# Turning moved ahead of the value products on TensorE, the whole copy ahead of the exponential on ScalarE

## What is computed

```python
scores = scale * np.matmul(q, k.transpose(0, 1, 3, 2))
thresh = np.max(scores, axis=-1, keepdims=True) - tau
scores = np.where(scores >= thresh, scores, -1000000000.0)
attn = np.exp(scores - np.max(scores, axis=-1, keepdims=True))
attn = attn / (np.sum(attn, axis=-1, keepdims=True) + 1e-09)
x = np.matmul(attn, v)             # then, heads side by side:
x = (h * np.tanh(softplus(h))) @ w_out    # h = x @ w_in
x = (h * clip(h + 3, 0, 6) / 6) @ w_out2  # h = x @ w_in2
```

## Time and profile before

| | |
|---|---|
| median of 3 runs | 1116.96 us (1115.6 to 1117.17) |
| the profiled execution, its own time | 1116.74 us |
| its span in the trace | 1115.0 us |
| attention stage | the first 310 us or so |
| PE busy | 1098.8 us, 99% of the span |
| VectorE busy | 423.6 us, 38% |
| ACT busy | 489.9 us, 44% |
| POOL busy | 263.5 us, 24% |

### The profile page before, as it was taken

The page is one execution under the profiler, slowest core; times in us unless marked ns, Lnnn a source line. Parts: engine busy times, 40 slices in busy tenths (PEclk is TensorE's granted clock), DMA queues, the critical chain, the costliest instruction groups (busy, mean ns, idle before and its releaser), DMA issues.

```text
span 1115.0 us, 15233 instructions
## 1 busy us (share of the span) xinstructions
PE 1098.8 (99%) x6064; PEld 880.3 (79%) x6064; DVE 423.6 (38%) x903; ACT 489.9 (44%) x882; POOL 263.5 (24%) x179
## 2 busy tenths in 40 slices
PE   6999999999999999999999999999999999999998
PEld 5767676767668888889988888888888888888897
DVE  6878887878831211112121112123223223222222
ACT  5778787877743332223232234442233233232232
POOL 6686558556621300000000015430000000000000
PEclk9999999999999999999999999999999999999999
DMA  7432223223022000000000022300010010010010
GB/s 221 132 108 65 77 74 97 65 66 96 11 76 76 1 1 1 1 1 1 1 1 1 19 75 96 96 18 1 1 38 1 1 38 0 1 39 1 1 39 20
DMA packets 42488, 46.09 MB, mean 41 GB/s; under 512 B 3504, under 2 KB 30128, under 8 KB 42416
## 3 DMA queue, kind: packets, MB, share of 16 engines
q1 hardware_dynamic: 42416, 45.10, 13.6%
HBM read 40.37 MB, written 4.72 MB: 40 GB/s over the span
## 4 chain that ended last, share of the span: by engine, by line
PE 97%; DVE 1%; ACT 1%; issue 1%; DMA 0%; SPq 0%; DVEq 0%
PE banks L489 35%; PE banks L462 12%; PE banks L464 12%; PE banks L463 12%; PE banks L409 8%; PE banks L356 7%; PE banks L368 5%; PE banks L364 3%; PE banks L389 2%; DVE probs L709 0%; DVE neg_max L725 0%; ACT exps L572 0%; DMA q_raw<-qT 0%; ACT probsT L537 0%; DVE totals L741 0%
## 5 line engine op out<-in xcount | busy, mean ns | idle before, releaser
L770 DVE SCALAR_TENSOR_TENSOR g_low<-gate,g_high 128x512 fp32r<-128x512 f32 (+1 forms) x160 | 102.7, 642 | 473.2 <-ACT g_high L645 473.2
L462 PE MATMUL banks<-x_low,w_in_high 128*128 128x512 f32 (+1 forms) x640 | 235.9, 369 | 0.0
L463 PE MATMUL banks<-x_high,w_in_low 128*128 128x512 f32 (+1 forms) x640 | 235.5, 368 | 0.0
L464 PE MATMUL banks<-x_high,w_in_high 128*128 128x512 f32 (+1 forms) x640 | 235.5, 368 | 0.0
L645 ACT ACTIVATE g_high<-gate 128x512 fp32r<-128x512 f32 (+1 forms) x160 | 94.3, 589 | 309.6 <-PE banks L489 309.1
L462 PEld LDWEIGHTS banks<-x_low,w_in_high 128*128 128x128 f32 x640 | 120.6, 188 | 21.2 <-issue 0.6
L463 PEld LDWEIGHTS banks<-x_high,w_in_low 128*128 128x128 f32 x640 | 120.6, 188 | 20.5
L464 PEld LDWEIGHTS banks<-x_high,w_in_high 128*128 128x128 f32 x640 | 120.7, 189 | 20.0
L725 DVE TENSOR_REDUCE neg_max<-banks 128x1 f32<-128x576 f32 x144 | 108.7, 755 | 50.3 <-PE banks L356 50.1
L489 PE MATMUL banks<-g_low,w_out_high 128*128 128x512 f32 (+1 forms) x320 | 118.0, 369 | 0.8 <-issue 0.8
L489 PE MATMUL banks<-g_high,w_out_low 128*128 128x512 f32 (+1 forms) x320 | 117.8, 368 | 0.0
(11 more groups left out here) (59 smaller groups left out, 1430.1 us busy)
## 6 DMA issues: line engine op xcount, KB each, us to landing
q_raw<-qT SPq DMA_DIRECT2D x64, 144.0 KB, 2.8
k_raw<-kT SPq DMA_DIRECT2D x64, 144.0 KB, 2.8
w_in_raw<-w_in SPq DMA_DIRECT2D x16, 512.0 KB, 4.3
w_out_raw<-w_out SPq DMA_DIRECT2D x16, 512.0 KB, 4.7
out<-x SPq DMA_DIRECT2D x18, 256.0 KB, 2.9
values<-v SPq DMA_DIRECT2D x16, 256.0 KB, 3.1
values<-v SPq DMA_DIRECT2D x16, 32.0 KB, 2.8
tau_in<-tau SPq DMA_DIRECT2D x1, 0.5 KB, 2.8
```

Of the source, the lines that this page charges most:

```text
L462: nc.tensor.matmul(bank, w_in_high[:, t, cols], low, start=(t == 0), stop=False)
L463: nc.tensor.matmul(bank, w_in_low[:, t, cols], high, start=False, stop=False)
L464: mm = nc.tensor.matmul(bank, w_in_high[:, t, cols], high, start=False, stop=(t == KT - 1))
L770: nc.vector.scalar_tensor_tensor(out=g_low[:, f % 2, 0:width], in0=gate[:, f % 2, 0:width], scalar=1 / 6 if layer_of(c) else 1.0, in1=f32( ...
```

## The change

In PE's `attention_step` the call of `turn` moves from the end to a place ahead of `spread_sums` and `mix`, right behind `score_tile`. In ACT's `attention_step` `keep_main` moves from behind the exponential to a place ahead of it, right behind `keep_tail`. The waits inside the functions stay as they are. VectorE's, POOL's and SP's programs are the same.

```diff
@@ PE attention_step @@
                 pair, b = it * PAIRS_IT + p - 1, (p + 1) % 2
+                if (not first or s >= 2) and (ahead or s < 2):
+                    turn(t - 2, (s - 2) % TILES_IT)
                 if not first or p == 1:
                     if i in (2, 3):
                         spread_sums(pair, b, i - 2)
...
                 if not first and i in (0, 1):
                     mix(it, pair - 1, 1 - b, 1, part1[i])
-                if (not first or s >= 2) and (ahead or s < 2):
-                    turn(t - 2, (s - 2) % TILES_IT)
@@ ACT attention_step @@
                 if (not first or s >= 2) and (ahead or s < 2):
                     keep_tail(t - 2, (s - 2) % TILES_IT, it * PAIRS_IT + (s - 2) // PAIR_TILES)
+                if (not first or s >= 2) and (ahead or s < 2):
+                    keep_main(t - 2, (s - 2) % TILES_IT)
                 if ahead:
                     act.wait_ge(max_ready, t + 1)
...
-                if (not first or s >= 2) and (ahead or s < 2):
-                    keep_main(t - 2, (s - 2) % TILES_IT)
```

## The result

The changed kernel takes 1163.14 us (four runs, 1162.98 to 1163.21) against 1116.98 us (1115.6 to 1117.17): 1.0416 times, with a 95% interval of 1.0398 to 1.0434. That is 46.2 us slower. The forecast was 1147 us, so its sign and place were right and its size was two thirds of what came (30.2 of 46.2 us).

The account below looks back on a forecast made before the run. PE, busy nearly throughout, was taken to bound the kernel, so its stalls in attention add one for one: 9.5 + 9.7 + 11.0 = 30.2 us on 1116.74 gives 1147 us, range 1132 to 1167 (own range 1138 to 1160).

Parts of the forecast that it names:

- (a): Steps 6 to 7: turning waits for weigh, queued behind scale_mixed on VectorE; 0.63 us in 15 pairs, 9.5 us.
- (b): Steps 1 to 2: turning waits for weigh behind the 320-column scale_mixed; 0.69 us in 14 pairs, 9.7 us.
- (c): Steps 2 to 4: scores wait for keep_tail behind the spread copy, main transposes for keep_main; 0.73 us, 15 pairs, 11.0 us.
- switches: Gaps between kinds of PE matmul around product blocks: value 0, bounds -0.09 to +0.13 us a step (-12 to +18 us).
- rival 1: Both ends of each product block: early weight loads save 0.22 us a step; 1117 or 1106 us; chance 0.06.
- (d): The other steps: weigh lets PE go at 1.65 us, PE returns at 1.90; no stall, cover 0.25 us.
- (e): The first pair and the end of attention: 0 us for the two together, from -2 to +1 us.
- Rival 2: Attention steps: ACT is not late, so only (a) and (b) appear; 1136 us; chance 0.15.
- Rival 3: Turning into product has the whole 0.22 us as gap, or (d)'s cover breaks by 0.3 us; 1165 us; chance 0.13.
- Rivals 1 and 4: The fourth: waits on scale_mixed shorter than read, ACT's hidden, front gap of product blocks saved; 1124 us; chance 0.06.

Follow-up runs that it names:

- The copy late: The changed kernel with the copy of the spread factors moved behind keep_tail and keep_main in ACT's queue: 1145.23 us, ratio 1.0255 to the kernel before.
- scale_mixed late: The changed kernel with scale_mixed moved behind weigh and the threshold in VectorE's queue: 1145.1 us, ratio 1.0255 to the kernel before.
- with the addition left out on both sides: Addition of 1e-9 to the row sums (L741) left out of the changed kernel, 1162.13 us, and of scale_mixed late, 1139.86 us.
- the run with both moves and no addition: The changed kernel with scale_mixed behind weigh, the spread copy behind keep_main, and the addition of 1e-9 (L741) left out: 1121.87 us, ratio 1.0054.
- ACT's half alone: The kernel before with only keep_main moved ahead of the exponential on ACT, PE as before: 1116.7 us, ratio 1.0002.
- scale_mixed late without the addition: The changed kernel with scale_mixed behind weigh and the addition of 1e-9 to the row sums (L741) left out: 1139.86 us, ratio 1.0212.

## Why the prediction was right in kind and short in size

Per pair the forecast was 30.2 / 15 = 2.0 us, the period shows 3.10 us. By the forecast's own steps, read from start to start, for the pair from 202.94 to 225.11 us of the changed kernel:

| step of the forecast | forecast, us a pair | measured |
|---|---|---|
| (a) turning waits in step 7 | 0.63 | 0.70 |
| (b) turning waits in step 2 | 0.69 | 0.75 |
| (c) scores wait for keep_tail, step 3 | 0.47 | 0.46 |
| (c) the same, step 4 | 0.25 | 0.25 |
| (c) main transposes wait for keep_main | 0.08 | 0.14 |
| (c) wait that was there before | -0.07 | -0.07 |
| restarts after the five waits | 0 | 0.41 |
| switches, nine steps | 0 | 0.46 |
| sum | 2.05 | 3.10 |

**The waits.** (a) and (b) were right in their releases: 1.39 us after the products' end was forecast and measured, and for (a) 1.33 and 1.33. What was off is the other side of the subtraction, the time at which PE comes back. I put 0.70 us for the scores, which is their length up to a product. Ahead of a turning they take 0.64, so PE came sooner and waited more. The 0.06 us that the switch saves in front went straight into the stall. (c) was right to 0.01 in both halves of the scores' wait. Its third part is 0.14 us where 0.08 was put: bank 6 was given as free at 1.41 us, though 0.79 + 0.57 is 1.36 and the text names nothing for the other 0.05; it was let go at 1.45 (207.57 to 209.02). The experiments bear the table out once restarts are added to the bare waits. The copy late should give 0.85 + 0.27 = 1.12 us a pair, 16.8 us in 15, and with the 0.16 us of every second pair some 18; 17.9 came. scale_mixed late should give 1.45 + 0.14 = 1.59 us a pair, some 23 us; with the addition left out on both sides 22.3 came (1162.13, then 1139.86), with it 18.

**Restarts,** a term that was missing. After a wait for keep_tail the next score matmul follows 0.24 us later and not 0.13 (208.40 to 208.64): 0.11 twice. A turning that waited takes 0.70 us up to the next block and not 0.63 (206.29 to 206.99): 0.07 twice, and 0.05 after the main transposes' wait. A wait on PE costs its length and then the start of a new group. The kernel before showed it for scores: behind the ones at 21.28 the next started at 21.52, 0.24 later, and I took only the release from that row. The turning at 25.30 can't show it, since its main transposes waited too.

**The switches** were the term with bounds of -0.09 and +0.13 us a step and 0 as its value. The turning costs 0.11 more ahead of a product, where 0.09 was put. The scores cost 0.06 less, where 0.09 was counted: the gap behind them shrinks from 0.22 to 0.14, but the first one takes 0.24 to the next behind a product where it was 0.22. Together 0.05 a step by the rows, 5.6 us by the run with both moves and no addition. The sign that I had named for a mis-sized switch, a distance from the turning to the product far from 0.45 us, did not say from which transpose: it is 0.63 from the first and 0.52 from the second. Why the boundary costs what it does stays open. The weight row ahead of the products shows 0.17 us idle for issue after a turning too (214.47), so rival 1, in which loads are drawn ahead there, did not come. By the rule of the Trainium skill (TensorE: Matmul & The Clock Gate, Part 2) such loads are drawn ahead when the row groups don't conflict or when they go to the background buffer; by that rule, the trace doesn't agree at this switch, unless neither condition holds there, which no run here shows.

**The cover of (d)** held for weigh, thin as it was: in the changed kernel steps 8, 0 and 1 are 0.05 or 0.06 us longer each and no more, and so is step 5 in every second pair. In the others it is 0.21 us longer, by keep_main and not by weigh. It is the cover of weigh that the collision with POOL breaks when scale_mixed stands late. (e) was about right: the spreading of the first pair starts 0.55 us later (28.45, then 29.00), within the bounds given; the other half of it, the end, was not read apart.

**The rivals.** Rival 2, ACT not late, fell with the waits for L553 and the 18 us that the later copy gives back. Rival 3 came near by its time (1165 us) but for another reason: not one dear switch but small terms in all nine steps, restarts among them. Rivals 1 and 4 did not come. That 1163 us lie inside the range of 1132 to 1167 is in part luck: they lie above the forecast's own 1138 to 1160, and the range reaches higher only for rival 3, whose mechanism was not the one.

None of the versions of this order that were run beats the kernel before. With the waits taken out of it 5.6 us are left for the switches.

## What to carry to other kernels

When a block on a full engine is moved, reckon each consumer from a common point: when is its data released, what stands ahead of it in its queue, and when does the full engine come back for the result. The danger is a small instruction that waits for the moved block (scale_mixed, the spread copy) with something urgent queued behind it; moving that one behind the urgent work gave back 38 of 46 us here. Give each wait on PE its restart as well, and take the length of a block up to the block that will really follow it.

## What the runs showed of the hardware

A nine-column SBUF-to-SBUF addition on VectorE (L741) takes 0.16 or 0.17 us alone. Where it comes while a POOL operation on SBUF has some time to run it lasts until 0.02 to 0.04 us after that one's end, up to 1.25 us behind one of 1.42 us (scale_mixed late, 151.88) and 1.27 behind one of 3.61 us (kernel before, 293.62); begun just ahead of one (ACT's half alone, 64.45 and 64.46) it took 0.16. The reciprocal over the same nine columns kept 0.20 to 0.22 us in every run, also when begun under a POOL operation (scale_mixed late without the addition, 108.58 under 108.36 to 109.78), and with the addition left out the long pairs shrank by 0.77 us. That the two engines meet at an SBUF interface is not shown by these runs. The Trainium skill, GPSIMD Engine Reference (Specifications), says that POOL shares its SBUF interfaces with VectorE, with contention for VectorE instructions in a 2-port perf mode or with two SBUF inputs. L741 has one SBUF input, and no run here shows in which mode it works; the trace agrees in that it took 1.23 against 0.16 us.

On PE a switch has a price on either side that depends on both neighbours: scores of 0.64 us ahead of a turning and 0.70 ahead of products, a turning of 0.52 between products and scores and 0.63 between scores and products. A wait adds a restart to its length, 0.11 us in scores and 0.05 to 0.07 in a turning.
